# A fused retention, channel-mix and sparse-attention kernel: 64-wide retention states in quarters of TensorE's array, and one GpSimd weighing moved

## What is computed

```python
# retention: per head, gamma = 1 - 2**(-5-h)
state = gamma * state + outer(k_t, v_t)
y_t = q_t @ state / 8
# channel mix
xn = (y - mean) / sqrt(var + 1e-6) * g_ln
x = y + relu(xn @ w_ch1) @ w_ch2
# 4 attention experts, each token weighted with its best 2
ye = softmax_causal(x wq[e], x wk[e]) @ (x wv[e]) @ wo[e]
out = sum over the two chosen e of w_e * ye
```

## Time and profile before

| | |
|---|---|
| median of 3 runs | 453.54 us (453.53 to 454.02) |
| profiled execution | 453.5 us, span 451.8 us |
| busy: PE / DVE / ACT / POOL | 444.0 / 321.2 / 220.5 / 292.5 us |
| TensorE's granted clock | 1.00 of full speed until the last microseconds |
| retention (first to last state output) | to about 60 us |
| the last two cycles of attention | about 418 to 442 us |

### The profile page before, as it was taken

How to read it: one execution, slowest core, us unless ns; L and a number is a source line. 1 busy time by engine, 2 the same in 40 slices (tenths; PEclk the granted TensorE clock), 3 DMA queues, 4 the chain that set the end, 5 groups by cost and what they waited for, 6 DMA issues and landing times.

```text
span 451.8 us, 8177 instructions
## 1 busy us (share of the span) xinstructions
PE 444.0 (98%) x2872; PEld 402.8 (89%) x2872; DVE 321.2 (71%) x669; ACT 220.5 (49%) x519; POOL 292.5 (65%) x391
## 2 busy tenths in 40 slices
PE   7999999999999999999999999999999999999997
PEld 6899998898898889889898988988999999999875
DVE  4565989668775767787776687658557878887853
ACT  3346737514532445552345145214436777777753
POOL 3766944978689499996966786641803355556650
PEclk9999999999999999999999999999999999999999
DMA  9999403222211203321121260020163543333214
GB/s 214 241 234 262 132 0 102 85 64 76 93 45 51 65 30 94 93 91 51 49 93 47 69 176 14 0 48 1 25 149 79 140 98 94 96 96 77 89 48 163
DMA packets 76520, 41.48 MB, mean 92 GB/s; under 512 B 48064, under 2 KB 70592, under 8 KB 76480
## 3 DMA queue, kind: packets, MB, share of 16 engines
q1 hardware_dynamic: 73824, 40.37, 33.2%
q10 hardware_dynamic: 2656, 0.60, 0.6%
HBM read 28.37 MB, written 3.15 MB: 70 GB/s over the span
## 4 chain that ended last, share of the span: by engine, by line
PE 91%; DVE 2%; SPq 2%; POOL 1%; DMA 1%; issue 1%; ACT 0%; POOLq 0%
PE ps L910 30%; PE ps L893 24%; PE ps L1015 8%; PE ps L1034 5%; PE ps L1068 4%; PE ps L1049 4%; PE ps L985 4%; PE ps L1092 3%; PE ps L766 2%; PE ps L753 2%; PE ps L773 2%; PE ps L743 2%; DMA raw_q<-in_q 1%; SPq L518 1%; PE ps L800 1%
## 5 line engine op out<-in xcount | busy, mean ns | idle before, releaser
L1276 ACT ACTIVATE h_t_hi<-ps 128x384 fp32r<-128x384 f32 x64 | 31.5, 492 | 128.4 <-DVE ps L1613 68.1
L910 PE MATMUL ps<-w_hi,h_t_lo 128*128 128x512 f32 x192 | 76.2, 397 | 0.0
L910 PE MATMUL ps<-w_lo,h_t_hi 128*128 128x512 f32 x192 | 75.8, 395 | 0.0
L910 PE MATMUL ps<-w_hi,h_t_hi 128*128 128x512 f32 x192 | 75.2, 392 | 0.0
L640 POOL TENSOR_TENSOR w_lo<-raw_w,w_hi 128x512 fp32r<-128x512 f32 x32 | 44.6, 1417 | 45.9 <-ACT w_hi L1224 40.5
L706 POOL TENSOR_SCALAR a<-a,inv_den,weight 128x768 f32<-128x768 f32 (+5 forms) x48 | 34.0, 718 | 52.9 <-DVE inv_den L1854 26.6
L1594 DVE SCALAR_TENSOR_TENSOR h_t_lo<-ps,h_t_hi 128x384 fp32r<-128x384 f32 x64 | 35.6, 557 | 32.6 <-ACT h_t_hi L1276 32.6
L619 POOL TENSOR_TENSOR w_lo<-w_sum,w_hi 128x256 fp32r<-128x256 f32 x60 | 44.5, 753 | 2.5
L910 PEld LDWEIGHTS ps<-w_hi,h_t_lo 128*128 128x128 f32 x192 | 36.0, 187 | 7.7
L893 PE MATMUL ps<-xq_T_lo,w_hi 128*128 128x384 f32 x120 | 40.6, 338 | 0.0
L1355 ACT ACTIVATE a<-a,neg_max 128x768 f32<-128x768 f32 (+5 forms) x48 | 32.3, 676 | 16.5 <-DVE neg_max L1835 16.5
(11 more groups left out here) (183 smaller groups left out, 1190.8 us busy)
## 6 DMA issues: line engine op xcount, KB each, us to landing
raw_w<-in_moe_w_ch SPq DMA_DIRECT2D x64, 256.0 KB, 2.8
k_twice_hi<-pj_hi SPq DMA_DIRECT2D x32, 96.0 KB, 2.2
k_twice_lo<-pj_lo SPq DMA_DIRECT2D x32, 96.0 KB, 2.2
out_y<-out_sb SPq DMA_DIRECT2D x12, 256.0 KB, 2.0
raw_k<-in_k SPq DMA_DIRECT2D x7, 384.0 KB, 5.0
raw_q<-in_q SPq DMA_DIRECT2D x7, 384.0 KB, 5.6
raw_v<-in_v SPq DMA_DIRECT2D x7, 384.0 KB, 4.1
q_both<-pj_hi SPq DMA_DIRECT2D x16, 96.0 KB, 2.1
```

What stands on the lines that cost most here:

```text
L910: mm = pe.matmul(acc_bank(tau), h_tile(a_, m, which)[:, u * P:(u + 1) * P], w2[b_][:, m % 2, part, :], start=(m % NG == 0 and which in ("1 ...
L1276: act.activation(h_tile("hi", m, part), part_bank(m, part), ACT.Relu).then_inc(s_hhi, 1)
```

## The change

State blocks become 128x64: head j has partitions 64j to 64j+63, and both heads the same 64 columns. The zeroed halves, their memset and semaphore go, and the key-values fit in bank 6. The state outputs become two 64x64 matmuls per chunk, one per head. For one group of each iteration (`crossed`: group 1, in the last iteration group 0) head 0's y goes to partitions 64 to 127 and head 1's to 0 to 63, in the chunk outputs too; ScalarE puts them back with two copies of 64x384. The state outputs of both groups stand in one step, in the order of chunks 1, 4, 2, 5, 3, and wait for the chunk outputs by a new semaphore; those of the last two iterations are interleaved per chunk. The first mean's bank is now apart from the key-values' bank, and the second mean comes behind all state outputs. In attention's last two cycles GpSimd does weigh(3c+2) between the two z-splits; waits are adapted.

```diff
-                state = sb(r, "state", [P, 2, NC - 1, P])
+                state = sb(r, "state", [P, 2, NC - 1, D])
...
         def first_mean_bank():
-            return ps[:, 7, P:P + W]
+            return ps[:, 7, 0:W]
         def kv_bank():
-            return ps[:, 6:8, :].rearrange("p a n -> p (a n)")[:, 0:(NC - 1) * P].rearrange("p (c e) -> p c e", c=NC - 1)
+            return ps[:, 6, 0:(NC - 1) * D].rearrange("p (c e) -> p c e", c=NC - 1)
+        def head_rows(j):
+            return slice(j * D, (j + 1) * D)
+        def crossed(it, g):
+            return (g == 1) != (it == NIT - 1)
+        def y_rows(it, g, j):
+            return head_rows(1 - j if crossed(it, g) else j)
...
@@ GpSimd
-                            pool.wait_ge(s_zlo, 2 * ((g - 2) // G))
+                            pool.wait_ge(s_zlo, 2 * ((g - 2) // G) - (g % G == 2 and g // G >= HALVES - 2))
...
-                if top == 0:
-                    pool.wait_ge(s_weighed, min(2 * LAST, 2 * (G * (n // 2 + 1) + 2)))
+                if top == 0 or n // 2 + 1 >= HALVES - 2:
+                    pool.wait_ge(s_weighed, min(2 * LAST, 2 * (G * (n // 2 + 1) + 2 + top)))
...
                 if c > 0:
                     z_split(2 * c - 2)
+                if 0 < c < HALVES - 2:
                     z_split(2 * c - 1)
                 weigh(G * c + 2)
+                if c >= HALVES - 2:
+                    z_split(2 * c - 1)
...
@@ TensorE
-                        pe.matmul(y_bank(it, g)[rows_, c * P:(c + 1) * P], raw["v"][:, it % RB, j, G * g + c], prob[:, it % 2, g, j, c, :],
-                                  start=(c == 0), stop=(g == 0 and c == 0), skip_group_check=True)
-            def state_outputs(it, g):
-                pe.wait_ge(s_st, (NC - 1) * it + G * g + G - 1)
+                        mm = pe.matmul(y_bank(it, g)[y_rows(it, g, j), c * P:(c + 1) * P], raw["v"][:, it % RB, j, G * g + c],
+                                       prob[:, it % 2, g, j, c, :], start=(c == 0), stop=(g == 0 and c == 0),
+                                       skip_group_check=True)
+                mm.then_inc(s_within, 1)
+            def add_state(it, c):
+                g = c // G
+                for j in range(2):
+                    mm = pe.matmul(y_bank(it, g)[y_rows(it, g, j), c % G * P:(c % G + 1) * P], state[head_rows(j), it % 2, c - 1, :],
+                                   q_t[head_rows(j), it % 2, c, :], start=False, stop=True, skip_group_check=True)
+                if c == G - 1 or c == (NC - 1 if it >= NIT - 2 else G):
+                    mm.then_inc(s_y, 1)
+            def state_outputs(it):
+                pe.wait_ge(s_within, 2 * it + 2)
+                pe.wait_ge(s_st, (NC - 1) * (it + 1))
+                for c in (1, 4, 2, 5, 3):
+                    add_state(it, c)
+            def last_state_outputs(g):
+                pe.wait_ge(s_within, 2 * NIT - 2 + 2 * g)
+                pe.wait_ge(s_st, (NC - 1) * (NIT - 1) + G * g + G - 1)
                 for c in range(max(1, G * g), G * g + G):
-                    mm = pe.matmul(y_bank(it, g)[:, (c - G * g) * P:(c - G * g + 1) * P], state[:, it % 2, c - 1, :],
-                                   q_t[:, it % 2, c, :], start=False, stop=True, skip_group_check=True)
-                mm.then_inc(s_y, 1)
+                    for it in (NIT - 2, NIT - 1):
+                        add_state(it, c)
...
-            for it in (NIT - 2, NIT - 1):
-                chunk_outputs(it, 0)
-            for it in (NIT - 2, NIT - 1):
-                state_outputs(it, 0)
-            for it in (NIT - 2, NIT - 1):
-                chunk_outputs(it, 1)
-            state_outputs(NIT - 2, 1)
+            for g in range(2):
+                for it in (NIT - 2, NIT - 1):
+                    chunk_outputs(it, g)
+                last_state_outputs(g)
             first_mean(1)
-            state_outputs(NIT - 1, 1)
...
@@ ScalarE, y_out
-                act.activation(x[:, it, G * g:G * g + G, :].rearrange("p c t -> p (c t)"), y_bank(it, g),
-                               ACT.Copy).then_inc(s_yx, 1)
+                if crossed(it, g):
+                    for j in range(2):
+                        copy = act.activation(x[head_rows(j), it, part_of(g), :],
+                                              y_bank(it, g)[head_rows(1 - j)].rearrange("p (c t) -> p c t", c=G), ACT.Copy)
+                else:
+                    copy = act.activation(x[:, it, part_of(g), :], y_bank(it, g).rearrange("p (c t) -> p c t", c=G), ACT.Copy)
+                copy.then_inc(s_yx, 1)
...
@@ VectorE
-            dve.memset(kv_bank(), 0.0).then_inc(s_zeros, 1)
```

More of the change, by code:

```diff
@@ L226, in retention_moe_program @@
         s_t, s_turned = sem("s_t"), sem("s_turned")
-        s_zeros, s_kv, s_st = sem("s_zeros"), sem("s_kv"), sem("s_st")
+        s_kv, s_st = sem("s_kv"), sem("s_st")
         s_s, s_prob = sem("s_s"), sem("s_prob")
-        s_y, s_yx = sem("s_y"), sem("s_yx")
+        s_within, s_y, s_yx = sem("s_within"), sem("s_y"), sem("s_yx")
         s_w1raw = [sem(f"s_w1raw{n}") for n in range(2)]
@@ L764, in chunk_outputs @@
                     for j in range(2):
-                        rows_ = slice(j * D, (j + 1) * D)
-                        pe.matmul(y_bank(it, g)[rows_, c * P:(c + 1) * P], raw["v"][:, it % RB, j, G * g + c], prob[:, it % 2, g, j, c, :],
-                                  start=(c == 0), stop=(g == 0 and c == 0), skip_group_check=True)
-            def state_outputs(it, g):
-                pe.wait_ge(s_st, (NC - 1) * it + G * g + G - 1)
+                        mm = pe.matmul(y_bank(it, g)[y_rows(it, g, j), c * P:(c + 1) * P], raw["v"][:, it % RB, j, G * g + c],
[17 more added lines that the diff above has]
+                pe.wait_ge(s_st, (NC - 1) * (NIT - 1) + G * g + G - 1)
                 for c in range(max(1, G * g), G * g + G):
-                    mm = pe.matmul(y_bank(it, g)[:, (c - G * g) * P:(c - G * g + 1) * P], state[:, it % 2, c - 1, :],
-                                   q_t[:, it % 2, c, :], start=False, stop=True, skip_group_check=True)
-                mm.then_inc(s_y, 1)
+                    for it in (NIT - 2, NIT - 1):
+                        add_state(it, c)
             def first_mean(b):
                 pe.wait_ge(s_const, 5)
-                if b == 0:
-                    pe.wait_ge(s_st, (NC - 1) * (HP + 2))
+                if b == 1:
+                    pe.wait_ge(s_xc, KT)
                 pe.wait_ge(s_acc, (HP - 1) * (b + 1))
@@ L792, in key_values @@
                     pe.wait_ge(s_st, (NC - 1) * it)
-                else:
-                    pe.wait_ge(s_zeros, 1)
-                if it == HP + 2:
-                    pe.wait_ge(s_xc, KT)
                 for c in range(NC - 1):
                     for j in range(2):
-                        rows = slice(j * D, (j + 1) * D)
-                        mm = pe.matmul(kv_bank()[rows, c, rows], scaled["k"][:, it % RB, c, rows], raw["v"][:, it % RB, j, c],
-                                       start=True, stop=True)
+                        mm = pe.matmul(kv_bank()[head_rows(j), c], scaled["k"][:, it % RB, c, head_rows(j)],
+                                       raw["v"][:, it % RB, j, c], start=True, stop=True)
                 mm.then_inc(s_kv, 1)
@@ L816, in _ @@
                 turn(1, unit)
-            for g in range(2):
-                state_outputs(0, g)
+            state_outputs(0)
             for it in range(1, NIT - 1):
@@ L827, in _ @@
                 if it > 1:
-                    for g in range(2):
-                        state_outputs(it - 1, g)
+                    state_outputs(it - 1)
                 for unit in range(4):
@@ L1861, in z_add @@
                 if n >= 2:
-                    dve.wait_ge(s_zlo, n - 1)
+                    dve.wait_ge(s_zlo, n if n == 2 * HALVES - 2 else n - 1)
                 dve.tensor_tensor(z_sum[rows, n % 2, :], bank[0:D], z_low[0:D, n % 2, :],
```

## The result

The kernel after takes 454.86 us (median of 20 executions, 453.74 to 456.45), the kernel before 453.49 (20 executions, 452.79 to 455.21). **The ratio is 1.0028, with a 95% interval of 1.0019 to 1.0037: slower by about 1.3 us.** The prediction had said 452.2, and faster. 454.86 lies above its range too.

A forecast was written before the change was run, and what follows sets the result against it. TensorE was taken as the bound, with ScalarE last by about 0.1 us in retention's steady iteration. 453.5 - 0.15 (retention) - 1.1 (weighing) = 452.25, rounded to 452.2 us; range 451.2 to 454.4.

The forecast's parts named there:

- The state step on TensorE: Retention's state outputs: twenty 64x64 instructions, four at once, take 0.91 us up to the transposes instead of 1.22.
- The evictions on ScalarE: Retention loop: y's extra copy takes back TensorE's gain; scores 2.76 us after state outputs start (T), before 2.73; +0.1 over three iterations.
- iterations longer than 6.6: Retention loop: a sign that the prediction is wrong, read as no quarters running at once; 6.4 us was expected.
- The mean iteration and the one behind it: Retention: TensorE is last and gains 0.3 us in the first mean's iteration; the next scores come level with before, total 0.
- Level with before: Retention, scores after the first mean's iteration: ScalarE does w1's scaling and splits without a gap, so 0 change.
- The last iterations: Retention's end: interleaved state outputs -0.35, chunk outputs +0.05, group 1's states +0.05; second mean moves by -0.25 us.
- The weighing: Attention's last two cycles: GpSimd's earlier third weighing removes TensorE's waits, gaining 0.26 + 0.83 = 1.1 us; bounds 0.3 and 1.1.
- (a): Rival, retention's evictions: crossed copies cost less in the chain, TensorE last at T + 2.3 to 2.4; 450.9 us, chance 0.10.
- (b): Rival, state outputs: quarters sharing a bank don't run at once; in pairs 454.3 us, chance 0.14; singly near 462, 0.04.
- (c): Rival, attention's end: another wait (low part or reciprocal) replaces the weighing's, leaving half of 1.1; 452.8 us, chance 0.14.

The follow-up runs named there:

- e10_not_crossed: e4_second_y_behind with no half of y crossed: only the two diagonal quarters, single copies of 128 partitions; 454.20 us, ratio 1.0012 to the kernel before.
- e3_straight_halves: The kernel after with y's uncrossed copy also split into two straight copies of 64 partitions; 457.92 us, ratio 1.0099 to the kernel before.
- e1_weigh_only: The kernel before with only GpSimd's new order and the waits that belong to it; 452.11 us, ratio 0.9977 to the kernel before.
- e4_second_y_behind: The kernel after with y's second (crossed) copy moved behind the transposed k and q on ScalarE; 451.33 us, ratio 0.9953 to the kernel before.
- e11: e4_second_y_behind with 17 more idle transposes on TensorE near the start; 451.54 us, ratio 0.9956 to the kernel before.
- e8_weigh_y_behind: e1_weigh_only with y's second half evicted behind the four turned copies, without quarters; 452.12 us, ratio 0.9974 to the kernel before.
- e9_no_warmup: e4_second_y_behind without the 18 idle transposes at the start; 452.73 us, ratio 0.9989 to the kernel before.

## Why the prediction was wrong

**The state step on TensorE: right.** Twenty instructions with 0.91 to the transposes were predicted, 0.82 measured, for 1.22 before. Four run at once at the slot of one (e10_not_crossed). The change of shape and the exposed load together come to 0.16 rather than the 0.25 taken.

**The evictions on ScalarE: the step that failed.** Its first half was right: y's first copy at T + 0.70, as measured. Then the prediction took 0.37 from each copy to the next "back to back" and put the scores at T + 2.76; they came at T + 3.15. The 0.37 had been read off copies of 128 partitions, y, k_t and q_t. For copies of 64 partitions it looked up only the length of one, 489 ns, which is the same, and did not read their *spacing*. Three boundaries touch the pair, at 0.13 more each: 0.4 per iteration. The rows were there to be read. ScalarE in attention of the kernel before:

```profile
429.96 0.49 ACT L1374 ACTIVATE z_low<-ps 64x384 f32<-64x384 f32 x1 [0.17 <-PE ps L1068]
430.47 0.88 ACT L1366 ACTIVATE a_low_hi<-ps 128x512 fp32r<-128x512 f32 x2
```

The copy of 64x384 starts at 429.96 and its successor, with no wait named, 0.51 later. With 0.51 in place of 0.37 three times the prediction's own sum gives T + 3.18, and three iterations at +0.45 each; measured were +0.42, +0.42 and +0.48, 1.3 us for the 0.1 predicted. The prediction named iterations longer than 6.6 as its sign that the quarters don't run at once; they came at 6.73 to 6.88 with the quarters at full pace, so the sign stood for the wrong cause.

The Trainium skill bears on this: ScalarE: Activation LUTs, "What ACT_TABLE_LOAD costs", says of a tile of 128 partitions that activations back to back overlap by about 93 ns. The rows agree for 128 partitions (0.49 long, 0.37 to 0.39 apart). For 64 the page says nothing, and the rows have no overlap (0.49 long, 0.50 apart, e3_straight_halves).

**The mean iteration and the one behind it: wrong, mostly by the same cause.** Predicted was -0.3 and then back to level, 0 for the two; measured were -0.12 and +0.85, +0.73. In the iteration with the mean ScalarE comes last (0.15 wait for q_t), so only 0.12 is gained. It also ends that iteration later behind the scores than before, and goes into w1's scaling and the splits with no gap. ScalarE before, then after:

```profile
48.04 1.56 ACT L1203 ACTIVATE xq_B_hi<-centred 128x768 fp32r<-128x768 f32 x2
49.64 0.49 ACT L1185 ACTIVATE x<-ps 128x384 f32<-128x384 f32 x1
50.31 0.49 ACT L1185 ACTIVATE x<-ps 128x384 f32<-128x384 f32 x1 [0.18 <-PE ps L773]
```

```profile
50.17 1.56 ACT L1227 ACTIVATE xq_B_hi<-centred 128x768 fp32r<-128x768 f32 x2
51.64 0.47 ACT L1209 ACTIVATE x<-ps 128x384 f32<-128x384 f32 x1
52.14 0.98 ACT L1206 ACTIVATE x<-ps 64x384 f32<-64x384 f32 x2
53.15 0.49 ACT L1198 ACTIVATE k_t<-ps 128x384 f32<-128x384 f32 x1
```

Before, y's second copy still waited 0.18 for TensorE; after, none waits. From the scores to y's first copy it is 4.33 before (45.31 to 49.64) and 4.73 after (46.91 to 51.64), from there to the next scores 1.98 and 2.43: +0.40 for the lag carried over and +0.45 for the copies make the +0.85. "Level with before" was wrong because here ScalarE was last and then had a full queue, and so kept its lag.

**The last iterations: right, by two misses that cancel.** -0.29 for -0.25. Group 0's states took 0.60 (0.75 predicted), the chunk outputs 1.60 (1.65), group 1's states 0.82 (0.8). The way to them from the last scores grew by 0.14 (3.82 for 3.68), for which there was no term; the states of group 0 gained 0.15 more than predicted.

**Nothing in attention ahead of its last cycles: a term that was missing.** Up to 0.6 us ahead of the first scores in the profiles of quarter kernels, 0.1 in the profile of after, and 0.3 behind them. It was not to be foreseen from the rows.

**The weighing: right in sum.** 1.1 us predicted, 1.2 in the profile of e1_weigh_only, 1.0 by its ratio, and 1.1 in the last two cycles of the kernel after. The split was not as predicted. From the first transposes of the last but one cycle to those of the last it is 11.36 before and 10.80 in e1_weigh_only (10.70 after), a gain of 0.56 for 0.26 predicted; the last cycle gained 0.56 for 0.83 (0.66 and 0.48 after).

**The rivals.** (a), crossed copies that cost less, was contradicted in the opposite direction: they cost more. But its picture of TensorE as last at T + 2.3 is what e4_second_y_behind realised by another edit, and its 450.9 was near the 451.33 measured there. (b), no four at once, did not happen (e10_not_crossed). Its number, 454.3, lies close to the result by accident: it had the state step at 1.35 and the last signal for ScalarE at T + 1.32, where the step took 0.82 and ScalarE was late by its own copies. (c) did not happen as priced; but VectorE's long addition delays its low part in the last but one cycle, and about 0.4 us of the weighing's possible gain goes there (e4 against e11). The missing rival was the plain one: a bound that lay 0.1 us behind TensorE, and a part with one more instruction for it. The prediction named that bound in its first paragraph, called the scores' start level at T + 2.76, and gave that price no range of its own.

Sum: 453.5 + 1.84 (for -0.15) - 1.1, + 0.1 to 0.6 ahead of attention's first scores and 0.3 behind them, gives 454.6 to 455.1; measured 454.86.

## What to carry to other kernels

Where two engines end level, price the second engine's added work by the start-to-start spacing of instructions *of the same form*, and not by an instruction's length or by the spacing of its larger likes. When a change shortens the leading engine's step, look at once at the order in the queue of the engine that comes last: here moving one copy behind the work that somebody waits for turned a loss of 1.3 us into a gain of 2.1. An engine that is last carries its lag through a stretch in which its own queue has no gap. When a profile differs from another before the changed work begins, look at several profiles first: here the start alone moved by 1.8 us from one to the next.

## What the runs showed of the hardware

- **ScalarE's copies of 64 partitions don't overlap with their neighbours.** 64x384 from PSUM, f32: 0.49 long, 0.50 to 0.51 from start to start, on both sides of each such copy; 128x384: 0.49 long and 0.37 to 0.39. Crossing the halves adds nothing (e3_straight_halves).
- **Four quarters of the array run at once, two of them on one PSUM bank.** Eight instructions of 64x64 by 128 columns start within 0.18 us; the step with its change of shape takes 0.82 for 1.24 in pairs. The Trainium skill, TensorEngine Tiling (Array Packing), "Restrictions and Gotchas", says that different row tiles cannot access the same bank at the same time; the runs here (other partitions of that bank for each tile) did not show that limit.
- **A two-element addition on VectorE took 1.03 us** (427.15) beside GpSimd's low split, which ran 1.01 us from 427.14, against 0.17 with no split beside it. The Trainium skill, SBUF — State Buffer, "Terms", says that VectorE and GpSimd share a pair of ports, held for a full instruction, and that the loser blocks. The traces agree: additions that start 0.01, 0.24 and 0.46 behind a split take 1.03 (after), 0.79 (e8_weigh_y_behind) and 0.58 (e1_weigh_only), and each ends 0.02 to 0.03 behind the split.
- **Without warm-up** three transposes took 0.87 us for 0.55 at the start (e9_no_warmup), while the granted clock is given as 1.00, the 2.4 GHz level, for that stretch. From 15.59 on the transposes take 0.55 again; TensorE had sat idle until 5.43. With the warm-up the profile of after still has six at 0.85 for three.
- **Single DMA issues on SyncE's queue took up to 1.9 us for 0.6** where a transfer of instructions on a DMA queue overlapped them (330.76 to 331.88 for the issue of 1.32 at 330.84 in after; all 37 issues of over 0.8 us in twelve profiles). The place moved with TensorE's instruction count.
